# Routed transformer block: the split schedule of the expert weights is reduced to what the next tile needs

## The reference

```
attention: B, H, S, D = 4, 8, 576, 64, block-causal mask with blocks of 64
x = attention output as [2304, 512]
x = (h - tanh(h)) @ w_out            with h = x @ w_in, w_in [512, 2048]

do_compute = x @ w_skip > 0          # tokens that pay for an expert
e_idx = argmax(x @ w_gate)           # one of 8 experts per token
for e in range(8):                   # w1 [8, 512, 1024], w2 [8, 1024, 512]
    h = max(xc[e_idx == e] @ w1[e], 0)
    y[e_idx == e] = gate_w * (h @ w2[e])
out[do_compute] = xc + y             # other tokens pass through unchanged
```

## Time and profile before

| | |
|---|---|
| median of three runs | 856.01 us (854.52 to 857.47) |
| time of the profiled execution | 856.01 us |
| its span, first to last instruction | 854.1 us |
| mean granted TensorE clock | 0.988 |
| PE busy | 817.5 us, 96% |
| DVE busy | 472.8 us, 55% |
| ACT busy | 316.8 us, 37% |
| POOL busy | 253.6 us, 30% |

### The profile page before, as it was taken

The page is one execution under the profiler, slowest core; times in us unless marked ns, Lnnn a source line. Parts: engine busy times, 40 slices in busy tenths (PEclk is TensorE's granted clock), DMA queues, the critical chain, the costliest instruction groups (busy, mean ns, idle before and its releaser), DMA issues.

```text
span 854.1 us, 18537 instructions
## 1 busy us (share of the span) xinstructions
PE 817.5 (96%) x5980; PEld 705.0 (83%) x5981; DVE 472.8 (55%) x1244; ACT 316.8 (37%) x831; POOL 253.6 (30%) x315
## 2 busy tenths in 40 slices
PE   5999999998999999999999999999988899999993
PEld 3555555557999999999999999999987688888882
DVE  4878788776644445444443444445457256665661
ACT  4676777661121121121211212112125145554550
POOL 4676666776800101001010010000111333333332
PEclk9999999999999999999999999999998999999998
DMA  8244434312301000000000000000042465556553
GB/s 183 57 109 109 109 89 108 98 45 76 99 1 29 1 0 28 0 18 9 0 28 0 9 19 0 28 0 7 23 159 93 136 220 170 189 204 208 185 175 110
DMA packets 83004, 66.80 MB, mean 78 GB/s; under 512 B 62970, under 2 KB 62970, under 8 KB 82960
## 3 DMA queue, kind: packets, MB, share of 16 engines
q1 hardware_dynamic: 77824, 60.56, 24.4%
q0 software_dynamic: 3952, 5.37, 1.9%
q10 hardware_dynamic: 1184, 0.30, 0.2%
HBM read 60.59 MB, written 8.82 MB: 81 GB/s over the span
## 4 chain that ended last, share of the span: by engine, by line
PE 89%; DMA 4%; DVE 3%; issue 1%; POOL 1%; ACT 0%; SPq 0%; POOLq 0%; DVEq 0%
PE psum L1238 64%; PE psum L1168 6%; PE psum L1146 6%; PE psum L1117 6%; PE psum L1102 2%; DMA w_half<-in_moe_w_dram 2%; PE psum L1274 2%; PE psum L1357 1%; PE psum L1282 1%; PE psum L1323 1%; DMA lists<-rec,slot_i 1%; DVE neg_max L782 1%; DMA q_rows<-in_q_dram 1%; DVE x_lo L830 0%; POOL probs L470 0%
## 5 line engine op out<-in xcount | busy, mean ns | idle before, releaser
L688 ACT ACTIVATE tanh_h<-psum 128x288 f32<-128x288 f32 x128 | 52.5, 410 | 312.7 <-PE psum L1238 312.7
L1238 PE MATMUL psum<-x_hi,wi_hi 128*128 128x288 f32 x512 | 154.7, 302 | 3.3 <-DVE x_lo L830 1.6
L1238 PE MATMUL psum<-x_lo,wi_hi 128*128 128x288 f32 x512 | 151.9, 297 | 0.0
L1238 PE MATMUL psum<-x_hi,wi_lo 128*128 128x288 f32 x512 | 151.6, 296 | 0.0
L1238 PE MATMUL psum<-g_hi,wo_lo 128*128 128x288 f32 x512 | 151.0, 295 | 0.0
L1238 PE MATMUL psum<-g_hi,wo_hi 128*128 128x288 f32 x512 | 151.0, 295 | 0.0
L1238 PE MATMUL psum<-g_lo,wo_hi 128*128 128x288 f32 x512 | 150.8, 295 | 0.0
L952 DVE TENSOR_TENSOR g<-psum,tanh_h 128x288 f32<-128x288 f32 x128 | 58.4, 457 | 141.6 <-ACT tanh_h L688 139.9
L494 POOL DMA_INDIRECT lists<-rec,slot_i x24 | 23.5, 980 | 371.2 <-DVE slot_i L887 322.8
L470 POOL TENSOR_SCALAR probs<-probs,row_inv 128x384 f32<-128x384 f32 (+2 forms) x96 | 97.7, 1028 | 59.1 <-DVE row_inv L789 59.1
L1238 PEld LDWEIGHTS psum<-x_hi,wi_hi 128*128 128x128 f32 x512 | 96.9, 189 | 4.2 <-issue 4.2
(11 more groups left out here) (184 smaller groups left out, 1305.3 us busy)
## 6 DMA issues: line engine op xcount, KB each, us to landing
w_half<-in_moe_w_dram SPq DMA_DIRECT2D x64, 512.0 KB, 4.1
q_rows<-in_q_dram SPq DMA_DIRECT2D x32, 144.0 KB, 3.0
out_dram<-x_rows SPq DMA_DIRECT2D x24, 192.0 KB, 2.1
k_rows<-in_k_dram SPq DMA_DIRECT2D x30, 144.0 KB, 3.1
v_rows<-in_v_dram SPq DMA_DIRECT2D x32, 128.0 KB, 2.3
w_raw<-in_moe_w_in_dram SPq DMA_DIRECT2D x16, 256.0 KB, 3.3
w_raw<-in_moe_w_out_dram SPq DMA_DIRECT2D x16, 256.0 KB, 2.6
v_rows<-in_v_dram SPq DMA_DIRECT2D x32, 16.0 KB, 2.2
```

The costliest lines, as they stand in the source:

```text
L688: act.activation(tanh_h[:, f % 2, :], h_ps[:, f % 2, 0:CH], ACT.Tanh).then_inc(tanh_done, 1)
L1238: mm = pe.matmul(dst, w, m, start=(first and n == 0), stop=(last and n == 2), skip_group_check=True)
```

## The change: the diff

Two of the four terms of the maximum and the limit by `2*last+2` are taken out. The table becomes

`tab_halves[0] = 2`, `tab_halves[j] = max(2e(j-1)+2, 2e(j)+1)`

It is written straight into the integer tile, so that the two scratch tiles `c_half` and `c_all` go and `tables` issues six instructions fewer. The thresholds `tab_free` and `tab_through`, the loads, and every loop are as they were.

```diff
-    c_half, c_all = sb("c_half", [1, NTAB], F32), sb("c_all", [1, 1], F32)
...
                 then(dve.tensor_scalar(c_h[:], c_e[:], 2.0, 2.0, ALU.mult, ALU.add))
                 then(dve.tensor_scalar(c_b[:], c_e[:], 2.0, 1.0, ALU.mult, ALU.add))
-
-                then(dve.memset(c_half[:], 2.0))
-                then(dve.tensor_tensor(c_half[:, 1:NTAB], c_h[:, 0:NTAB - 1], c_b[:, 1:NTAB], ALU.max))
-                then(dve.tensor_scalar(c_b[:], c_b[:], 2.0, None, ALU.add))
-                then(dve.tensor_scalar(c_h[:], c_h[:], 2.0, None, ALU.add))
-                then(dve.tensor_tensor(c_half[:, 2:NTAB], c_half[:, 2:NTAB], c_b[:, 0:NTAB - 2], ALU.max))
-                then(dve.tensor_tensor(c_half[:, 3:NTAB], c_half[:, 3:NTAB], c_h[:, 0:NTAB - 3], ALU.max))
-                then(dve.tensor_scalar(c_all[:], c_last[:], 2.0, 2.0, ALU.mult, ALU.add))
-                then(dve.tensor_tensor(tab_halves[:], c_half[:], c_all[:].to_broadcast([1, NTAB]), ALU.min))
+                then(dve.memset(tab_halves[:], 2))
+                then(dve.tensor_tensor(tab_halves[:, 1:NTAB], c_h[:, 0:NTAB - 1], c_b[:, 1:NTAB], ALU.max))
                 then(dve.memset(tab_free[:], 1))
                 then(dve.memset(tab_through[:], 1))
```

## The result

The changed kernel is slower: 862.28 us median of six runs (861.46 to 863.36) against 856.74 us (854.52 to 857.71) for the kernel before, a ratio of 1.0068 with a 95% interval of 1.0052 to 1.0086, or 4.5 to 7.4 us. The forecast was 859.3 with a range up to 862.2. The direction and the place were right, the size was not. The profiled execution took 863.56 us with a span of 861.9; it is the slowest of the changed kernel's seven executions on record. So the spans of the two profiles lie 7.8 us apart and the medians only 5.5.

A forecast was written before the change was run, and what follows sets the result against it. PE was taken to bound the kernel, with ACT, DVE, POOL and loads hidden in the loop. Span 854.1 plus a 3.3 us stall (2.7 to 4.5) plus 1.9 around it gave 859.3 us, range 857.6 to 862.2.

The forecast's parts named there:

- The table: Schedule of splits per iteration: entries go from 2 2 3 4 5 6 7 8 to 2 2 3 4 4 5 7 8.
- the empty iteration: Loop iteration 2, near 710.7 us, loses its half on ACT and DVE; nothing gained, as PE was not waiting there.
- the double split: Iteration 4, near 735.4 us, splits halves 5 and 6, sixteen pieces in one run on ACT and DVE.
- the single place of the stall: PE's one loop pause, ahead of `turn_he` and the first product after iteration 4's splits; 3.3 us (2.7 to 4.5).
- The six instructions: The shorter `tables` ahead of the loop frees 1.2 us on DVE, counted as no gain beside 2.68 us of idling.
- The pause between two halves: ACT in iteration 4: waits and two numbers read again before half 6, half of 2.50, 1.3 us.
- The load of half 6: Lands at 742.9, slowest 744.6, while ACT wants it at 745.0; so no delay in iteration 4.
- The late load of half 7: Lands near 755.2, ACT wants it at 754.35 and waits 0.9 us; hidden, as PE needs the results later.
- DVE's second half: DVE in iteration 4 starts half 6 at 746.0, takes 4.90 us and has it split at 750.9.
- I take the clock as kept: TensorE's clock does not fall in the new pause (2.1 us, eight transposes, 1.1 us); nothing added to the time.
- the rival with 0.28: TensorE's clock falls in the new pause, costing 1.75 us on top of the stall: 861.1 us; chance 0.28.
- The sum: Whole kernel: span 854.1 plus the 3.3 us stall, plus 1.9 us around it, gives 859.3 us.

The follow-up runs named there:

- e3: The changed kernel with its shorter table, filled by another formula that gives the old schedule for these inputs; 857.06 us, 1.0006 of before.
- e1: The kernel before without the term 2e(j-3)+4, the term 2e(j-2)+3 kept; 860.89 us, 1.0050 of before.
- e2: The kernel before without the term 2e(j-2)+3, the term 2e(j-3)+4 kept; 860.03 us, 1.0052 of before.
- e9: The changed kernel with its two unused scratch tiles kept, so later tiles lie at their old addresses; 862.21 us, 1.0066 of before.
- e4: The changed kernel with ACT reading its two thresholds ahead of the wait for the load; 861.46 us, 1.0060 of before.
- e6: The changed kernel with 24 extra transposes on PE ahead of `turn_he` in iteration 5; 861.71 us, 1.0043 of before.
- e8: The kernel of e2 with `he` and `xe` written between the first and second half on ACT and DVE; 864.33 us, 1.0069 of before.

## Why the prediction was right in kind and wrong in size

- **The table.** Right in every entry, and so were the empty iteration, the double split, and the single place of the stall.
- **The six instructions, "taken as nothing".** The shorter table was free (e3), as the 2.68 us of idling said.
- **The pause between two halves, 1.3 us.** This step failed, in two ways that hide each other. With the load in place the reading costs nothing (e1, e2): the sequencer reads while activations run. Where it comes out, the two numbers cost 1.7 us (the chain above, e9), not 1.3. In the changed kernel the pause was 2.32, 1.0 more than forecast, because the load was late and the reads stood behind it (e4). The constant 2.50 us of rows 3 and 4 were read as the price of reading; they are that only when ACT has nothing left to execute.
- **The load of half 6, "covered by 2.1 us, in the worst case 0.4".** This failed too. The cover was counted up to the first piece of half 6 (745.0), but ACT waits for the load ahead of its reads, which is from the end of half 5 (743.70) on. By the prediction's own numbers that leaves 0.8 us of cover at the median landing and makes the slowest (744.6) 0.9 late. And the load took longer. The first issue was at 734.03 and the last landing at 745.02, 11.0 us where 9.7 was worked out from a median landing of 4.1; the last piece alone took 5.0. The median over 64 pieces was too kind for a path with two of them in a row; why these were slow is open (that the gather and the scatter share their engines is only argued). The late load of half 7 was hidden as forecast (ACT stood 4.01 us ahead of it, PE did not).
- **DVE's second half, 4.90 us.** It took 5.32 beside POOL's copy, 0.4 us more. The same pair stands in e6 (5.32 with a copy of 1.08) and e8 (5.33 with 1.09).
- **"I take the clock as kept".** This was the largest single miss, 1.9 us, and it was the rival with 0.28. The pause that came was 3.14 us and not 2.1, and its eight transposes were already at the low clock. The rows had one fall and one not, and "more transposes within", the reason given for the clock to hold, did not hold it. Of the seven double-split kernels without extra work in the pause six fell and only e1 kept it; e2 and e4 fell with stalls of no more than 2.68 and 2.62 us, so even the lower end of the forecast stall was no safe case. In e6, with work in the pause, the cost was gone. The example of the Trainium skill ("TensorE: Matmul & The Clock Gate", Seeing it yourself) put the fall 5.2 us after the last matmul; here the clock fell about 2.7 us after the last dense work (748.51 to 751.2), and in e2 it fell within two pauses of 0.75 and 1.43 us with transposes between. The traces decide against it as a margin.
- **The sum.** Where 3.3 us were forecast, the loop lost 7.0: 4.8 of stall, 1.9 of clock, 0.3 of longer iterations that nothing in the prediction stood for. Of the 4.8, 3.3 are as forecast, 1.0 is the longer pause and 0.4 DVE's slower half.

## What to carry to other kernels

A look-ahead term in a schedule can be worth much more than the one step it moves: putting off one split also put off the load two halves on and queued two splits ahead of the small steps that TensorE needs next. Put reads of registers and thresholds ahead of the wait that may really stand, for behind it they come out in full. Where TensorE will pause for a microsecond or more, price the pause with the low clock behind it, and try idle transposes in it if a bank is free.

## What was not expected of the hardware

- ACT's sequencer can hide the reading of the two numbers of a half (1.7 us when exposed) behind running activations: 16 pieces in 8.45 us in e1.
- At pauses of this size the same length can end either way: e1 kept 1.00 through 0.70 and 1.43 us and e2 fell in 0.75 and 1.43, which made 24 matmuls 5.73 or 7.19 us. The 1.92 us behind the loop cost nothing in the kernel before and 1.6 us in the profiles of e1, e8 and e9.
- Moving tiles by 160 bytes on each partition made every iteration of the loop 0.02 to 0.03 us longer (12.34 to 12.37), and moving them back undid it (e9).
- 24 extra transposes in a pause of 3 us took 2.78 us of PE that nobody waited for; the 24 matmuls behind them took 5.71 us where the changed kernel's trace has 7.63.
